# Complex mixing from scaled fp16 parts in three products, in a fused Fourier-filter and feed-forward kernel

## The reference

```python
X = np.fft.rfft(x, axis=1)                       # over the 3008 tokens
Yr = Xr @ w_r - Xi @ w_i + b_r                   # complex mixing, 256 x 256
Yi = Xr @ w_i + Xi @ w_r + b_i
Yr, Yi = soft threshold of each by lam = 0.01
y = np.fft.irfft(Y, n=3008, axis=1)
h = y.reshape(12032, 256) @ w_in                 # to 2048 columns
P = a0 + a1 h + a2 h^2 + a3 h^3 ;  Q = 1 + |b0||h| + |b1| h^2
out = (P / (Q + 1e-6)) @ w_out                   # back to 256 columns
```

## Time and profile before

| | us |
|---|---|
| median of 3 runs | 1465.79 (1462.83 to 1466.27) |
| the profiled execution: time, span | 1461.36, 1459.6 |
| PE busy | 1409.4 (97%) |
| PEld busy (weight loads) | 1004.1 (69%) |
| DVE busy | 1260.0 (86%) |
| ACT busy | 1223.0 (84%) |
| POOL busy | 636.0 (44%) |

### The profile page before, as it was taken

The page is one execution under the profiler, slowest core; times in us unless marked ns, Lnnn a source line. Parts: engine busy times, 40 slices in busy tenths (PEclk is TensorE's granted clock), DMA queues, the critical chain, the costliest instruction groups (busy, mean ns, idle before and its releaser), DMA issues.

```text
span 1459.6 us, 20395 instructions
## 1 busy us (share of the span) xinstructions
PE 1409.4 (97%) x7008; PEld 1004.1 (69%) x7008; DVE 1260.0 (86%) x1462; ACT 1223.0 (84%) x1687; POOL 636.0 (44%) x420
## 2 busy tenths in 40 slices
PE   6998999999999999999999999999999999999986
PEld 2885677777777777777777777776766666666665
DVE  0355988889889889889899989989989999999997
ACT  3566888888888888889878888888879999999985
POOL 0000444445445444444445545444535555555555
PEclk9999999999999999999999999999999999999998
DMA  9876566656456655655555555555555555555443
GB/s 278 253 231 158 128 142 144 140 125 153 107 124 148 151 107 136 140 103 126 111 120 112 123 108 121 121 113 105 116 109 107 106 93 114 113 111 110 89 87 69
DMA packets 97830, 188.01 MB, mean 129 GB/s; under 512 B 11136, under 2 KB 57664, under 8 KB 97728
## 3 DMA queue, kind: packets, MB, share of 16 engines
q0 software_dynamic: 29952, 98.58, 36.9%
q1 hardware_dynamic: 67776, 88.12, 20.6%
HBM read 50.60 MB, written 37.49 MB: 60 GB/s over the span
## 4 chain that ended last, share of the span: by engine, by line
PE 71%; DVE 16%; issue 5%; ACT 5%; DMA 1%; POOL 1%; POOLq 0%; SPq 0%; ACTq 0%; DVEq 0%
PE h_ps L479 23%; PE o_ps L504 8%; PE o_ps L492 8%; PE o_ps L494 8%; DVE den L854 4%; DVE num L860 4%; PE d L426 4%; DVE g_hi L849 4%; PE d L427 4%; DVE num L867 4%; PE d L456 3%; PE d L433 3%; PE d L419 2%; PE d L413 2%; PE h_ps L426 2%
## 5 line engine op out<-in xcount | busy, mean ns | idle before, releaser
L913 POOL TENSOR_TENSOR g_lo<-num,sq 128x940 fp32r<-128x940 f32 (+1 forms) x208 | 462.0, 2221 | 132.3 <-DVE num L860 132.1
L905 POOL DMA_DIRECT2D den<-sq x208 | 182.4, 877 | 685.3 <-PE o_ps L504 394.5
L492 PE MATMUL o_ps<-g_hi,wout_hi 128*128 128x470 f32 (+1 forms) x832 | 344.8, 415 | 0.0
L494 PE MATMUL o_ps<-g_hi,wout_lo 128*128 128x470 f32 (+1 forms) x832 | 310.3, 374 | 0.0
L479 PE MATMUL h_ps<-yt_hi,win_hi 128*128 128x470 f16 (+1 forms) x832 | 301.3, 362 | 3.4 <-DVE num L872 3.4
L479 PE MATMUL h_ps<-yt_lo,win_hi 128*128 128x470 f16 (+1 forms) x832 | 299.8, 360 | 0.0
L479 PE MATMUL h_ps<-yt_hi,win_lo 128*128 128x470 f16 (+1 forms) x832 | 299.4, 360 | 0.0
L655 ACT ACTIVATE den<-h_ps,coef 128x940 f32<-128x940 f32 (+1 forms) x208 | 214.2, 1030 | 51.7 <-PE h_ps L479 48.2
L872 DVE SCALAR_TENSOR_TENSOR num<-num,coef,h_ps 128x940 f32<-128x940 f32 (+1 forms) x208 | 244.5, 1176 | 5.0
L849 DVE SCALAR_TENSOR_TENSOR g_hi<-num,a_sb,sq 128x940 fp32r<-128x940 f32 (+1 forms) x208 | 244.6, 1176 | 4.3 <-ACT sq L719 4.3
L504 PE MATMUL o_ps<-g_lo,wout_hi 128*128 128x470 f32 (+1 forms) x832 | 225.5, 393 | 23.5 <-POOL g_lo L913 23.3
(11 more groups left out here) (98 smaller groups left out, 1400.3 us busy)
## 6 DMA issues: line engine op xcount, KB each, us to landing
den<-sq POOLq DMA_DIRECT2D x200, 470.0 KB, 4.4
spec<-s1w SPq DMA_DIRECT2D x64, 192.0 KB, 3.1
z_in<-spec SPq DMA_DIRECT2D x96, 128.0 KB, 3.3
spec<-s_out SPq DMA_DIRECT2D x96, 128.0 KB, 3.3
xw<-in_x SPq DMA_DIRECT2D x31, 384.0 KB, 4.5
out_t<-o_sb SPq DMA_DIRECT2D x25, 470.0 KB, 4.7
zp_in<-spec SPq DMA_DIRECT2D x22, 480.0 KB, 4.7
inv_in<-in_inv SPq DMA_DIRECT2D x96, 64.0 KB, 2.3
```

Of the source, the lines that this page charges most:

```text
L492: pe.matmul(o_ps[:, h, 0:w], wout_hi[:, f, h * P:(h + 1) * P], g_hi[q % 3][:, j, 0:w], start=f == 0, stop=False)
L494: mm = pe.matmul(o_ps[:, h, 0:w], wout_lo[:, f, h * P:(h + 1) * P], g_hi[q % 3][:, j, 0:w], start=False, stop=False)
L913: pool.tensor_tensor(g_lo[r % 2][:, :, 0:cols(r)], ring(num, r), ring(sq, r), ALU.mult).then_inc(n_g, 1)
```

## The change

The mixing takes its operands in fp16 upper and lower parts, as f1 does: three products for each of the four fp32 matmuls of before, 12 passes of 256 columns. The weights are scaled by a power of two from their largest entries, the input by one per batch from the sum of the absolute values of `x`. These sums are new work: of s1 inputs 0 to 19 on DVE, of the others on ACT (`sum_abs`). `evacuate_s2` is one ACT copy with a scale; the lower part, and the negation of both parts, are now two DVE instructions (`lower`), on which s3 waits. `shifted` takes the scale back out. s4 is issued behind s3 and not ahead of the g_lo product. The first spectral s2, one s1 and the two s5 of tile 1 are issued ahead of slot 0, and requests for x are spread.

```diff
-EARLY_X = {u: S1N // 2 + 3 + i for i, u in enumerate((3, 5, 8, 11, 14))}
+EARLY_X = {u: S1N // 2 + 3 + i for i, u in enumerate((3, 5, 8, 11, 14, 20))}
+FIRST_X = {2: S1N + 1, 5: S1N + 2, 9: S1N + 3}
-S5_AT = {t * SLOTS + 1 + 2 * half: (t + 1) * KH + half for t in range(NT - 1) for half in range(KH)}
+S5_AT = {t * SLOTS + 1 + 2 * half: (t + 1) * KH + half for t in range(1, NT - 1) for half in range(KH)}
+X_AT = {1: 20, 2: 33, 3: 75}
+X_STEPS = 6
+FRONT_S1 = S1N + 4
+FIRST_SUMS = S1N - 4
...
             def step_s3(c, bank):
-                pe.wait_ge(e2, (c + 1) * 2)
+                upper, lower = xt[c % 2][:, 0], xt[c % 2][:, 1]
+                pe.wait_ge(e2l, c + 1)
                 for h in range(KH):
-                    pe.matmul(bank[:, 0:D], xt[c % 2][:, h, 64:192], wr_sb[:, h, :], start=h == 0, stop=False)
-                    mm = pe.matmul(bank[:, 0:D], xt[c % 2][:, h, 0:128], wi_sb[:, h, :], start=False, stop=h == 1)
+                    pe.matmul(bank[:, 0:D], upper[:, h, 64:192], wr_hi[:, h, :], start=h == 0, stop=False)
+                    pe.matmul(bank[:, 0:D], upper[:, h, 64:192], wr_lo[:, h, :], start=False, stop=False)
+                    pe.matmul(bank[:, 0:D], lower[:, h, 64:192], wr_hi[:, h, :], start=False, stop=False)
+                pe.wait_ge(e2n, c + 1)
+                for h in range(KH):
+                    pe.matmul(bank[:, 0:D], upper[:, h, 0:128], wi_hi[:, h, :], start=False, stop=False)
+                    pe.matmul(bank[:, 0:D], upper[:, h, 0:128], wi_lo[:, h, :], start=False, stop=False)
+                    mm = pe.matmul(bank[:, 0:D], lower[:, h, 0:128], wi_hi[:, h, :], start=False, stop=h == KH - 1)
                 mm.then_inc(p3, 1)
...
@@ tensor engine, behind group_f1(1)
+            pe.wait_ge(e4, PRE)
+            step_s2(PRE, d0[:, :])
+            step_s1(2 * S1N, d1[:, :])
+            pe.wait_ge(e5l, KH)
+            step_s5(2, o_ps[:, 0, :])
+            step_s5(3, o_ps[:, 1, :])
...
@@ ACT, evacuate_s2
-                act.activation(xt[c % 2][:, :, 64:192], both, ACT.Copy).then_inc(e2, 1)
-                act.activation(xt[c % 2][:, :, 0:64], both[:, :, 64:128], ACT.Copy, scale=-1.0).then_inc(e2, 1)
+                act.wait_ge(k_x, X_STEPS * (c // K2 + 1))
+                act.activation(xt[c % 2][:, 0, :, 64:192], both, ACT.Identity,
+                               scale=x_scale[:, c // K2:c // K2 + 1]).then_inc(e2, 1)
+            def sum_abs(g):
...
+                act.activation(x_size[0:ROWS, :], x_in[g // 2 % 4][:, at:at + 2, :].rearrange("r p d -> r (p d)"), ACT.Abs,
+                               accum_out=x_sum[0:ROWS, g:g + 1]).then_inc(x_act, 1)
...
@@ DVE
+            def lower(c, bank):
+                both = bank[:, 0:KH * P].rearrange("p (h m) -> p h m", h=KH)
+                dve.wait_ge(e2, c + 1)
+                dve.scalar_tensor_tensor(out=xt[c % 2][:, 1, :, 64:192], in0=both, scalar=x_scale[:, c // K2:c // K2 + 1],
+                                         in1=xt[c % 2][:, 0, :, 64:192], op0=ALU.mult, op1=ALU.subtract).then_inc(e2l, 1)
+                dve.wait_ge(e2l, c + 1)
+                dve.tensor_scalar(xt[c % 2][:, :, :, 0:64], xt[c % 2][:, :, :, 128:192], -1.0, None, ALU.mult).then_inc(e2n, 1)
...
@@ DVE, shifted
-                dve.tensor_tensor(t1[:, :], bank[:, 0:D], bias_sb[:, :], ALU.add).then_inc(m_t, 1)
+                dve.scalar_tensor_tensor(out=t1[:, :], in0=bank[:, 0:D], scalar=x_inv[:, c // K2:c // K2 + 1],
+                                         in1=bias_sb[:, :], op0=ALU.mult, op1=ALU.add).then_inc(m_t, 1)
...
@@ DVE, in the loop, between the two multiplications of slot q
+                if q == 0:
+                    lower(PRE, d0[:, :])
+                if q - 1 in S2_AT and q >= 2:
+                    lower(S2_AT[q - 1], d0[:, :])
```

181 lines of the change are left out of this document (151 added, 30 removed).

## The result

| | median us | runs | ratio to the kernel before, 95% interval |
|---|---|---|---|
| before | 1465.6 | 6 | |
| changed | 1472.0 | 6 | 1.0051 [1.0038, 1.0063] |

A forecast was written before the change was run, and what follows sets the result against it. TensorE was taken as the bound up to the last spectral slot, between 1060 and 1120 us. Loop 21, moved steps 4.5 and front 4 us sum to 29.5 us gained, forecast 1434 us, range 1421 to 1450.

The forecast's parts named there:

- The mixing, 0.41 us a step: TensorE's mixing: twelve fp16 passes take 1.31 us instead of 1.72, saving 0.41 us per step.
- (c): Rival: weight loads no longer hide in short fp16 passes, mixing takes 2.46 us, about 1530 us in all; chance 0.02.
- (d): Rival: the mixing gets no shorter because its passes stall on their waits, 1464 us; chance 0.06.
- I take 0.18, bounds 0.1 to 0.3: Time in us for VectorE's negation of 256 fp16 columns in each mixing step.
- The booking of 0.55 us per pair: VectorE's added work per spectral step, lower part and negation less overlap; 0.49 us per pair in the second window.
- The rooms: Margin per pair of slots before VectorE replaces TensorE as the bound: 0.65 us in the first window, 0.1 in the second.
- Where the lower part waits: Second multiplication 1.3 us late behind ScalarE's copy, absorbed by idle before `ythr`; 0.06 us per pair lost to slot 84, 0.16 after.
- the tighter consumer: GpSimd's g_lo, made from VectorE's remainder one slot after; TensorE asks for it 0.43 us sooner.
- Rival (a): VectorE becomes the bound in all spectral pairs, 13.38 us each, half the loop gain goes, 1446 us; chance 0.18.
- Rival (b): All present VectorE idle time survives with the new wait on top, 14.99 us a pair, 1537 us; chance 0.06.
- The moves, 4.5 us: Steps issued ahead of slot 0 fill TensorE's idle time there: net gain 2 to 7 us, taken as 4.5.
- The front, 4 us: Steps ahead of the loop: 8.6 us from shorter mixing in 21 steps, less deductions and a later start, gains 4.

The follow-up runs named there:

- low_n3: The changed kernel with the lower part and the negation moved behind the slot's second multiplication in the loop, both still on VectorE; 1452.7 us, 0.9922 of the kernel before.
- act_n3: The changed kernel with the negation on ScalarE and the lower part behind the second multiplication; 1446.0 us, 0.9878 of the kernel before.
- neg_act: The changed kernel with the negation moved from VectorE to ScalarE; 1452.8 us, 0.9925 of the kernel before.
- moves_only: The kernel before, fp32 mixing kept, with only the moved steps, the earlier x requests and the fourth step's new place; 1.0000 of the kernel before.
- no_neg: The changed kernel without its 96 negations, the negated columns filled once with a constant; 1449.6 us, 0.9907 of the kernel before.
- bare: The changed kernel without the negations, the 44 sums of magnitudes and the three later measuring chains; 1444.6 us, 0.9868 of the kernel before.
- act_yl: act_n3 with yt_lo placed behind the two VectorE operations that followed it; 1437.3 us, 0.9826 of the kernel before.

## Why the prediction was wrong, step by step

- **The mixing, 0.41 us a step: right.** 1.32 us for twelve passes against 1.31 forecast; rivals (c) and (d) did not occur. The Trainium skill's rule in "TensorE: Matmul & The Clock Gate", section "The mechanism", that loads overlap only on another row group, is not borne out: 0.11 us a pass, where an fp16 load takes 98 ns. The same section also lets a load into a background weight buffer go ahead, which the prediction left out, and with which the rows agree.
- **"I take 0.18, bounds 0.1 to 0.3", the negation: the step that failed.** It measured 0.23 alone and 0.39 on average, 0.62 behind 700 us. The booking of 0.55 us per pair came out as (375.83 - 353.23) / 29 = 0.78 in the first window, and 347.45 / 27 - 11.90 = 0.97 in the second where 0.49 was booked (0.88 between the starts of slots 86 and 138, where no part of a pair is left over). The rooms were 0.65 and 0.1. The 0.18 stood below the nearest row, 215 ns for half the columns, with no row for it (the estimate of 0.13 us beside it was further off still), and the hold was not thought of at all. The rest of the booking was small too: `lower` took 0.48 for 0.45 and the shift 0.47 for 0.42, so that even without a hold VectorE's work per pair grew by 0.68 and 0.56 us (low_n3, slots 26 to 84 and 86 to 138), already more than either room. What I could have seen stands in the kernel before: VectorE's third multiplication, both inputs from SBUF, 1.13 us long, lasts over 1.3 us in 12 of 208 places; here it ended at 900.81, 1.01 us behind a g_lo that ended at 899.80.

```profile
897.94 1.19 DVE L872 SCALAR_TENSOR_TENSOR num<-num,coef,h_ps 128x940 f32<-128x940 f32 x1
899.05 1.76 DVE L854 SCALAR_TENSOR_TENSOR den<-den,g_hi 128x940 f32<-128x940 f32 x1
```
```profile
897.29 2.51 POOL L913 TENSOR_TENSOR g_lo<-num,sq 128x940 fp32r<-128x940 f32 x1
```

- **Where the lower part waits: mechanism right, size too small.** The idles ahead of `ythr` and `yt_lo` gave way as forecast, but so did all the room: 0.06 and 0.16 us a pair were booked for it, and the lower part's new place measured 6.8 us in act_n3 against neg_act, the place of yt_lo behind it 8 us.
- **The way to the loss was named, its size was not.** The prediction called g_lo the tighter consumer, and one of its signs of being wrong was idle time of TensorE ahead of g_lo products; there were 10 such waits in the 29 pairs of the first window and 25 in the 27 of the second, 23 us in all. Of its other signs the idle ahead of `ythr` went as said, the passes came at 0.11 us, but the pair did not come down to 13.4 us, and VectorE was 94% busy in the first window, not over 95%.
- **Rival (a)** was the case that came, a vector engine that bounds, but its 13.38 us a pair lacked the hold; the pair is 13.81 between slots 26 and 84 (13.53 from 46 to 74, without the slow place at slot 40). It took half the loop's gain; in truth all went, and in the later slots more. It also did not let the later window turn negative.
- **Rival (b)** did not come: the old idles did not survive.
- **The moves, 4.5 us: wrong,** 0 +/- 1.3 us in moves_only.
- **The front, 4 us: wrong.** It lost 3.8. Without the negation it breaks even (no_neg), without the sums too it gains 2.1 (bare). The ring over ScalarE in the steps with a weight part was priced as the vector engine's work, 2.7 us, not as a ring of 3.11. That the ring is what costs is not shown: on the changed kernel the order that opens it gained 1.8 us, inside the intervals.
- **The scale's cost, 1.1 us in the front and nothing in the loop: too small,** 7 us.

The account, from 29.5 us forecast as gain to 7.5 lost, 37 in all: the negation 21, the sums and chains 7 (with it 27 of 37 in bare). The other 10 are not divided by a run. The moves are up to 4.5 of them, and 6.0 stand in slots 40 to 44 and 88 to 92 of bare; both fit the waits for the copy and for yt_hi that act_n3 and act_yl remove, which was not tried on bare.
